# Three fused stages on one core: pack of attention in two parts, W' emptied by ScalarE and stored per batch, join reordered with four early steps

## The reference

```python
batch, n_heads, seq, head_dim = (8, 8, 576, 64); n_pack = 32
p_packed = sm_attn(p, k, v)              # softmax attention of 32 rows p over 576 keys, per head
out = sm_attn(q, p_packed, p_packed)     # softmax attention of 576 rows q over the 32 packed rows
x = out.transpose(0, 2, 1, 3).reshape(4608, 512)
h = x @ w_in                             # 512 -> 2048
P = a[0] + a[1]*h + a[2]*h**2 + a[3]*h**3
Q = 1.0 + abs(b[0])*abs(h) + abs(b[1])*h**2
y = (P / (Q + 1e-6)) @ w_out             # 2048 -> 512
h = y @ w_in2                            # 512 -> 1024
solu = h * softmax(h)
ln = (solu - mean) / sqrt(var + 1e-6) * g_ln
return ln @ w_out2                       # 1024 -> 512
```

## Time and profile before

| | us |
|---|---|
| median of three runs (lowest, highest) | 1328.96 (1325.56, 1330.09) |
| the profiled execution, its own time | 1329.48 |
| its span in the profile | 1327.3 |
| attention without jobs, until | 79.9 |
| attention with jobs, until | 207 |
| join, until | 263.6 |
| rational stage, until about | 885 |
| last stage, until the end | 1327 |

### The profile page before, as it was taken

How to read it: one execution, slowest core, us unless ns; L and a number is a source line. 1 busy time by engine, 2 the same in 40 slices (tenths; PEclk the granted TensorE clock), 3 DMA queues, 4 the chain that set the end, 5 groups by cost and what they waited for, 6 DMA issues and landing times.

```text
span 1327.3 us, 27768 instructions
## 1 busy us (share of the span) xinstructions
PE 1221.9 (92%) x10944; PEld 1095.7 (83%) x10944; DVE 1009.8 (76%) x1694; ACT 862.3 (65%) x1406; POOL 306.9 (23%) x205
## 2 busy tenths in 40 slices
PE   5678776599999999999999999999999999999999
PEld 3455554499999999999999999998888888888887
DVE  3657666599999999999999999986555555555553
ACT  3345435489989899999999999974344343433433
POOL 2222222033323232333332333331110111001100
PEclk8899888699999999999999999999999999999999
DMA  7668865402121121211212121111111111111110
GB/s 267 218 232 313 283 225 187 161 26 75 43 67 43 42 75 44 66 59 36 66 60 75 38 73 40 36 35 51 48 47 32 47 47 47 46 33 47 47 33 32
DMA packets 69790, 114.28 MB, mean 86 GB/s; under 512 B 9264, under 2 KB 39984, under 8 KB 69680
## 3 DMA queue, kind: packets, MB, share of 16 engines
q1 hardware_dynamic: 69680, 112.75, 26.1%
HBM read 72.36 MB, written 40.37 MB: 85 GB/s over the span
## 4 chain that ended last, share of the span: by engine, by line
PE 46%; DVE 29%; issue 14%; ACT 11%; DMA 0%; POOL 0%; ACTq 0%; SPq 0%; DVEq 0%
DVE num L989 6%; DVE rec L986 6%; PE ps_h L72 6%; PE ps_h L74 6%; PE ps_h L73 6%; PE ps_o L72 5%; PE ps_o L74 5%; PE ps_o L73 5%; DVE den L978 4%; ACT rec L898 3%; DVE num L973 3%; PE ps_s L359 3%; ACT rec L901 3%; PE ps_t L1231 2%; PE ps_s L347 2%
## 5 line engine op out<-in xcount | busy, mean ns | idle before, releaser
L72 PE MATMUL ps_y<-g_hi,wout_hi 128*128 128x288 f32 x1024 | 306.7, 299 | 16.7 <-ACT y_out L930 16.7
L940 POOL TENSOR_TENSOR den<-den,h_abs 128x576 f32<-128x576 f32 x128 | 203.0, 1586 | 458.5 <-ACT den L893 458.5
L73 PE MATMUL ps_y<-g_lo,wout_hi 128*128 128x288 f32 x1024 | 304.7, 298 | 0.0
L74 PE MATMUL ps_y<-g_hi,wout_lo 128*128 128x288 f32 x1024 | 303.8, 297 | 0.0
L72 PEld LDWEIGHTS ps_y<-g_hi,wout_hi 128*128 128x128 f32 x1024 | 194.5, 190 | 19.9 <-issue 19.8
L74 PEld LDWEIGHTS ps_y<-g_hi,wout_lo 128*128 128x128 f32 x1024 | 195.3, 191 | 0.0
L73 PEld LDWEIGHTS ps_y<-g_lo,wout_hi 128*128 128x128 f32 x1024 | 194.8, 190 | 0.0
L72 PE MATMUL ps_h<-x_hi,wp_hi 128*128 128x288 f32 x512 | 154.7, 302 | 10.5 <-DVE wp_lo L955 10.5
L73 PE MATMUL ps_h<-x_lo,wp_hi 128*128 128x288 f32 x512 | 153.4, 300 | 0.0
L74 PE MATMUL ps_h<-x_hi,wp_lo 128*128 128x288 f32 x512 | 152.7, 298 | 0.0
L893 ACT ACTIVATE den<-h_abs,kept 128x576 f32<-128x576 f32 x128 | 111.4, 870 | 38.4 <-DVE rec L986 38.3
(11 more groups left out here) (120 smaller groups left out, 2623.1 us busy)
## 6 DMA issues: line engine op xcount, KB each, us to landing
wp_scratch<-wp_out SPq DMA_DIRECT2D x32, 512.0 KB, 4.0
wp_lo<-wp_scratch SPq DMA_DIRECT2D x128, 128.0 KB, 3.0
k_main<-in_k SPq DMA_DIRECT2D x16, 576.0 KB, 6.4
q_main<-in_q SPq DMA_DIRECT2D x16, 576.0 KB, 6.7
v_main<-in_v SPq DMA_DIRECT2D x16, 576.0 KB, 5.7
y_scratch<-y_out SPq DMA_DIRECT2D x16, 576.0 KB, 3.3
y_lo<-y_scratch SPq DMA_DIRECT2D x36, 256.0 KB, 3.0
out<-result SPq DMA_DIRECT2D x36, 256.0 KB, 2.1
```

Of the source, the lines that this page charges most:

```text
L72: pe.matmul(out, lh, rh, start=first, stop=False)
L73: pe.matmul(out, lh, rl, start=False, stop=False)
L74: return pe.matmul(out, ll, rh, start=False, stop=last)
L940: pool.tensor_tensor(den[s % 2][:, :, :], den[s % 2][:, :, :], h_abs[s % 2][:, :, :], ALU.mult)\
```

## The change

Six things are changed. The pack is issued in two halves with the transposes of q between them. Of the scores of q only the last of nine tiles waits for the low half of the packed transpose. Of the first 12 jobs, ACT empties both heads of a block in one instruction of 1024 elements, and DVE none; the last four jobs are shared as before. `wp_scratch` is laid out by batch, so that a store of 128 rows goes to four places of 32 rows, and a load of a block is one transfer of 128 rows in place of four of 32. The orders on ACT and DVE inside an iteration are changed (ACT splits the next weights ahead of the second exponential, DVE does the sums ahead of the normalised pack and turns the keys ahead of the low half). The join is reordered and holds four steps of the rational stage in place of three. The diff, cut to what is spoken of:

```diff
@@ -269,15 +273,16 @@
 
     def store_job(sp, m):
         quad, a, half = job_parts(m)
-        for r, ready in enumerate((wp_act_out, wp_dve_out)):
-            sp.wait_ge(ready, 2 * m + 2)
-            sp.dma_start(wp_d[quad, 2 * a + r, :, half * 2 * BLOCK:(half + 1) * 2 * BLOCK],
+        sp.wait_ge(wp_act_out, 2 * m + 2)
+        wait_for(sp, wp_dve_out, dve_blocks(m + 1))
+        for r in range(2):
+            sp.dma_start(wp_d[QUAD * quad:QUAD * (quad + 1), 2 * a + r, :, half * 2 * BLOCK:(half + 1) * 2 * BLOCK],
                          wp_out[m % 2][:, r, :, :].rearrange("p n f -> p (n f)")).then_inc(wp_stored[m % 2][r], 16)
 
     def store_a2(sp, i):
         bt, g = group_at(i)
         sp.wait_ge(a2_ready, i + 1)
-        sp.dma_start(a2_d[HEAD_TILES * bt + g], a2_out[i % 2][:, :]).then_inc(a2_stored[bt // QUAD], 16)
...
@@ -349,16 +354,18 @@
                                        start=(b == 0), stop=(b == DB - 1), skip_group_check=True)
             mm.then_inc(s1_done, 1)
 
-        def pack(pe, i):
-            pe.wait_ge(probs1T_ready, i + 1)
-            pe.wait_ge(v_in[i % 2], 16 * (i // 2 + 1))
-            wait_for(pe, shift2_ready, i)
-            wait_for(pe, packT4_lo_ready, i)
-            for t in range(RUN):
+        def pack(pe, i, half):
+            if half == 0:
+                pe.wait_ge(probs1T_ready, i + 1)
+                pe.wait_ge(v_in[i % 2], 16 * (i // 2 + 1))
+                wait_for(pe, shift2_ready, i)
+                wait_for(pe, packT4_lo_ready, i)
+            for t in range(half * PAIRS, (half + 1) * PAIRS):
                 for h in range(GH):
                     mm = pe.matmul(ps_pack[head(h), :], probs1T[head(h), t, :], v_main[i % 2][head(h), t, :],
                                    start=(t == 0), stop=(t == RUN - 1), skip_group_check=True)
-            mm.then_inc(pack_done, 1)
+            if half == 1:
+                mm.then_inc(pack_done, 1)
 
         def turn_queries(pe, i):
             pe.wait_ge(q_in[i % 2], 16 * (i // 2 + 1))
...
@@ -379,9 +385,10 @@
 
         def scores_of_q(pe, i):
             pe.wait_ge(packT2_out, i + 1)
-            pe.wait_ge(packT4_lo_ready, i + 1)
             pe.wait_ge(qT_out, i + 1)
             for j in range(PAIRS):
+                if j == PAIRS - 1:
+                    pe.wait_ge(packT4_lo_ready, i + 1)
                 for h in range(GH):
                     mm = pe.matmul(scores2[head(h), j * 2 * PACK:(j + 1) * 2 * PACK], qT[i % 2][:, j, head(h)],
...
@@ -408,33 +414,36 @@
         scores_of_packed(pe, 0)
         for i in range(GROUPS):
             if i >= 1:
-                pack(pe, i - 1)
+                pack(pe, i - 1, 0)
             turn_queries(pe, i)
             if i >= 1:
-                turn_packed(pe, i - 1)
+                pack(pe, i - 1, 1)
             job_block(pe, i, 0)
             if i >= 1:
+                turn_packed(pe, i - 1)
+            job_block(pe, i, 1)
+            if i >= 1:
                 scores_of_q(pe, i - 1)
-            job_block(pe, i, 1)
             if i + 1 < GROUPS:
                 scores_of_packed(pe, i + 1)
 
         last = GROUPS - 1
-        pack(pe, last)
+        pack(pe, last, 0)
+        pack(pe, last, 1)
         job_block(pe, GROUPS, 0)
-        turn_packed(pe, last)
         pe.wait_ge(exp1_ready, GROUPS)
         features(pe, 0)
+        turn_packed(pe, last)
+        job_block(pe, GROUPS, 1)
         scores_of_q(pe, last)
-        job_block(pe, GROUPS, 1)
+        pe.wait_ge(wp_act_out, 2 * job_at(GROUPS) + 1)
+        features(pe, 1)
         a, b, c, d = range(JOBS - LAST_JOBS, JOBS)
         last_job_block(pe, a, 0)
-        features(pe, 1)
+        features(pe, 2)
         last_job_block(pe, a, 1)
-        last_job_block(pe, b, 0)
-        last_job_block(pe, b, 1)
-        features(pe, 2)
-        for m in (c, d):
+        features(pe, 3)
+        for m in (b, c, d):
             for n in range(2):
                 last_job_block(pe, m, n)
 
...
+                wait_for(act, wp_stored[m % 2][1], 16 * (m // 2))
+                act.activation(wp_out[m % 2][:, :, n, :], ps_turn[:, 2 * n:2 * n + 2, :], ACT.Copy)\
+                    .then_inc(wp_act_out, 1)
+            else:
+                act.activation(wp_out[m % 2][:, 0, n, :], job_bank(m, n, 0), ACT.Copy).then_inc(wp_act_out, 1)
+
+        weights_high(act, 0)
         for i in range(GROUPS):
-            weights_high(act, i)
             first_terms(act, i)
             last_pair_to_sbuf(act, i)
+            qT_to_sbuf(act, i)
             if i == 1:
                 act.wait_ge(zeros, 1)
             if i >= 1:
                 packT_to_sbuf(act, i - 1)
-            qT_to_sbuf(act, i)
             if job_at(i) is not None:
                 job_to_sbuf(act, job_at(i), 0)
+                job_to_sbuf(act, job_at(i), 1)
+            if i + 1 < GROUPS:
+                weights_high(act, i + 1)
+            else:
+                next_coefficients(act)
+                first_splits(act)
             if i >= 1:
                 second_terms(act, i - 1)
-            if job_at(i) is not None:
-                job_to_sbuf(act, job_at(i), 1)
 
         last = GROUPS - 1
-        next_coefficients(act)
-        first_splits(act)
+        a, b, c, d = range(JOBS - LAST_JOBS, JOBS)
         job_to_sbuf(act, job_at(GROUPS), 0)
+        step(act, 0)
         packT_to_sbuf(act, last)
-        step(act, 0)
+        job_to_sbuf(act, job_at(GROUPS), 1)
         second_terms(act, last)
-        job_to_sbuf(act, job_at(GROUPS), 1)
-        a, b, c, d = range(JOBS - LAST_JOBS, JOBS)
+        step(act, 1)
         job_to_sbuf(act, a, 0)
-        step(act, 1)
         job_to_sbuf(act, a, 1)
         job_to_sbuf(act, b, 0)
+        step(act, 2)
         job_to_sbuf(act, b, 1)
-        step(act, 2)
-        for m in (c, d):
-            for n in range(2):
-                job_to_sbuf(act, m, n)
+        job_to_sbuf(act, c, 0)
+        step(act, 3)
...
@@ -597,47 +615,43 @@
         turn_keys(dve, 0)
         for i in range(GROUPS):
             row_max(dve, i)
+            if i >= 2:
+                second_sums(dve, i - 2)
             if i >= 1:
                 normalized_pack(dve, i - 1)
-            if i >= 2:
-                second_sums(dve, i - 2)
             turn_probs1(dve, i)
+            if i + 1 < GROUPS:
+                turn_keys(dve, i + 1)
             if i >= 1:
                 packT_low(dve, i - 1)
-            if i + 1 < GROUPS:
-                turn_keys(dve, i + 1)
             if i >= 2:
                 turn_probs2(dve, i - 2)
-            if job_at(i) is not None:
-                job_to_sbuf(dve, job_at(i), 0)
             if i >= 1:
                 shifted_scores(dve, i - 1)
-            if job_at(i) is not None:
-                job_to_sbuf(dve, job_at(i), 1)
 
         last = GROUPS - 1
-        normalized_pack(dve, last)
-        second_sums(dve, last - 1)
+        a, b, c, d = range(JOBS - LAST_JOBS, JOBS)
         next_coefficients(dve)
         first_splits(dve)
-        job_to_sbuf(dve, job_at(GROUPS), 0)
+        second_sums(dve, last - 1)
+        normalized_pack(dve, last)
+        step(dve, 0)
         packT_low(dve, last)
         turn_probs2(dve, last - 1)
-        step(dve, 0)
         shifted_scores(dve, last)
-        job_to_sbuf(dve, job_at(GROUPS), 1)
-        a, b, c, d = range(JOBS - LAST_JOBS, JOBS)
+        step(dve, 1)
         job_to_sbuf(dve, a, 0)
         second_sums(dve, last)
-        step(dve, 1)
         job_to_sbuf(dve, a, 1)
+        job_to_sbuf(dve, b, 0)
+        step(dve, 2)
         turn_probs2(dve, last)
-        job_to_sbuf(dve, b, 0)
         job_to_sbuf(dve, b, 1)
-        step(dve, 2)
-        for m in (c, d):
-            for n in range(2):
-                job_to_sbuf(dve, m, n)
+        job_to_sbuf(dve, c, 0)
+        step(dve, 3)
+        job_to_sbuf(dve, c, 1)
+        job_to_sbuf(dve, d, 0)
+        job_to_sbuf(dve, d, 1)
 
     def gpsimd(pool, step):
...
+    EARLY = 4
...
@@ -762,19 +776,18 @@
 
     def load_x(sp, q):
         bt, half = q // 2, q % 2
-        sp.wait_ge(attention["a2_stored"][0 if q == 0 else 1], 16 * HEAD_TILES * QUAD)
+        for stored in attention["a2_stored"][0 if q == 0 else 1]:
+            sp.wait_ge(stored, 16 * QUAD)
         sp.dma_start(x_raw(q), a2_d[HEAD_TILES * bt:HEAD_TILES * (bt + 1), :, half * CHUNK:(half + 1) * CHUNK]
                      .rearrange("g p n -> p g n")).then_inc(x_in[q % 2], 16)
 
     def load_block(sp, bt, n):
-        quad, at = bt // QUAD, (bt % QUAD) * PACK
+        quad = bt // QUAD
         for stored in attention["wp_stored"]:
             for r in range(2):
                 sp.wait_ge(stored[r], 16 * (JOBS // 4) * (quad + 1))
-        for h in range(GH):
-            sp.dma_start(block_raw(n)[h * PACK:(h + 1) * PACK, :, :],
-                         wp_d[quad, h:HEADS:GH, at:at + PACK, n * BLOCK:(n + 1) * BLOCK].rearrange("g r f -> r g f"))\
```

(58 more changed lines are left out.)

1 line of the change is left out of this document (removed).

## The result

The changed kernel takes **1365.8 us** (median of 4 runs, 1365.09 to 1367.45) where the kernel before takes 1328.56: 37 us slower, ratio 1.0285, 95% interval 1.0264 to 1.0305. The profiled execution took 1365.09 us, 35.6 more than that of before.

A forecast was written before the change was run, and what follows sets the result against it. Before 263.6 us a ring of waits bounds the loop, with DMA close behind; the changed stores, on four engines, become the bound. 1329.5 + 34.8 (first x) + 9.1 (join), about +44, gives 1373.5 us; range 1340 to 1412.

The forecast's parts named there:

- Stores on four engines: Stores of W': each, cut 4 x 32, was to run on four of 16 DMA engines at 25.0 GB/s each.
- First x +34.8 us: Job loop: 4.12 MB on each of four engines delays the rational stage's first split of x by 34.8 us.
- Join +9.1 us: Join: the second x, queued behind the last stores, is split 71.7 us after the first instead of 62.6.
- Low half only at the last tile: Scores of q on PE: waiting for the low half only at the last tile costs nothing and gives nothing.
- The other parts, -4 in the loop and -7 in the join, hidden: Loop and join: reordering gains 4 us and 7 us, hidden while the stores of W' come last.
- The DVE chain of 1.78 us: Job iterations: one copy (0.61 us) and the second softmax sums (1.17 us) leave DVE's 7.6 us chain.
- the transposes' 1.03 us: Job iterations: nine transposes of q inside the pack delay its end by 1.03 us.
- The weights' 4 us: Job loop: ACT's earlier wait for weights takes half of the remaining 0.75 us gain per iteration, leaving 4 us.
- A: Rival, stores of W': they run on 16 engines as before, giving 1318.5 us; chance 0.12.
- B: Rival, stores of W': four engines at about 30 GB/s each, loss and gain cancel, 1328 us; chance 0.03.
- C: Rival, stores of W': four engines at 28.2 GB/s each throughout, giving 1347 us; chance 0.05.
- D: Rival, job loop: waits for the single weights buffer do not overlap transfers, iterations 18.2 us, total 1385 us; chance 0.10.

The follow-up runs named there:

- e2: The kernel before with only the new layout of W' (stores cut 4 x 32, one-piece block loads, attention output semaphores per buffer): 1369.16 us, ratio 1.0314.
- e1: The changed kernel with the old layout of W' (stores of 128 rows outermost, block loads in four pieces), all other parts kept: 1315.65 us, ratio 0.9908.
- e3: The changed kernel with its layout by batch, but each store of W' issued as four pieces of 32 rows: 1313.36 us, ratio 0.9892.
- m1: Transfers only, 512 KB one at a time in several shapes, no kernel: 128 rows 2.6 us, 4 x 32 10.0 us, four pieces of 32 rows 3.5 us.
- e8: e1 with the scores of q waiting for the low half of the pack ahead of their first tile again: 1327.74 us, ratio 0.9995.
- e7: e1 with DVE's old order (second softmax sums behind the normalised pack, keys turned behind the low half): 1319.29 us, ratio 0.9925.
- e12: e1 with the W' blocks of the eleven jobs inside the loop emptied by ACT and DVE in halves again: 1313.25 us, ratio 0.9886.
- e5: e1 with the pack in one piece again, ahead of the transposes of q: 1311.21 us, ratio 0.9873.
- e6: e1 with the weights split by ACT at the start of an iteration again, behind the second exponential: 1312.43 us, ratio 0.9881.
- e9: e1 with three early steps, step 3 of the rational stage behind the jobs again: 1318.67 us, ratio 0.9929.
- e10: e3 with the first of each job's two stores as one transfer cut 4 x 32 again: 1327.85 us, ratio 1.0001.

## Why the prediction was right, point by point

*Stores on four engines: right.* e2 and e1 show that this part makes the loss, e3 that the counting does and not the address, m1 the four engines. The Trainium skill's rule on the slowest dimension ("DMA: Bandwidth & Descriptors", section "Why a DMA increments its semaphore by 16 and not by 1") gives 4 for this store, and the traces agree: four small packets for a store of 4 x 32, a share of 0.2 and some 100 GB/s where only stores of 4 x 32 are left, 0.90 and 298 GB/s with pieces of 32 rows.

*First x +34.8 us: right in kind, 9.3 too high.* Measured +25.5. Two terms of the product were off. The first store is issued at 75.85 us instead of 81.14, because the light iterations became shorter. The 4.12 MB then land in about 161 us instead of 164.9: 25.6 GB/s per engine over the stretch where I took 25.0 (26.1 in a steady iteration, which takes 16.3 us where 17.0 were forecast). The isolated store was the right row to take, its highest slot (28.2) and the share among 16 (21.0) were not. The "~27 GiB/s" of the Trainium skill, in the table at the head of "DMA: Bandwidth & Descriptors" (29.0 GB/s), is more than the 26.1 of the steady iteration.

*Join +9.1 us: right.* From split to split 73.56 us against the 71.7 of the working, +10.95, with ACT waiting for the second x as forecast, 12.42 us. The sum is 7.7 us too high (1373.5 against 1365.8), mostly by the first term; that this one is 1.9 us too low hides a part of it.

*Low half only at the last tile, "costs nothing and gives nothing": wrong.* It was judged from VectorE's rows alone. The wait stood on PE, 1.7 us before the scores in a light iteration of before. The clock of that run of scores is the last shown under e8:

```profile
62.39 2.15 PE L386 MATMUL ps_s<-packT,qT 128*32 128x64 f32 x72 [1.70 <-issue]
```

e8 shows 12 us for it. By the seventh copy of the queries, the last one before the job iterations settle, 9.2 us of them are there (86.38 us in e8, 77.16 in e1, 88.17 in the kernel before). For the light iterations the prediction had put the other parts at nothing too. It came out right all the same because the stores hide this gain but for the 5.3 us by which they start earlier.

*The other parts, -4 in the loop and -7 in the join, hidden:* the sum of 11 is near the 12.5 us of e1, but it is made of other terms, and the nearness is luck. In e1's trace 11.0 us are gained by the seventh copy of the queries; from there to the last copy e1 takes 116.1 us where the kernel before takes 114.0, so the job iterations, forecast at -4, gain nothing. The DVE chain of 1.78 us an iteration (e7 and e12 gave +3.6 and -2.4 where 17.8 were summed) is worth little, and the transposes' 1.03 us less than said (e5: -4.4 where -10 was forecast, and not told from no change); the likely reason, not tried by itself, is that the job iterations wait for transfers too (share 0.90 in e3). The weights' 4 us (e6: 3.2) and the early step's 4 us (e9: 3.0) fit, without being told from no change. From split to split the join takes 59.2 us in e1, 3.4 less than before; 1.5 us more come from the negation (ACT waits 1.41 us for it where the earlier trace rows have 2.92).

*Rivals.* A's time, 1318.5, is near that of e1 and e3 (1315.7 and 1313.4), where the stores are on 16 engines. Its 188.7 us are those in which the changed kernel would equal the one before; with 11 us gained they would be 177.7, at 32.7 GB/s for each of the four. B (30.8 GB/s) and C (28.2) are out by the 25.6 measured. D is out: its chain of weights is the one that the profile names, but the period is 16.3, not 18.2, and e2 has the same period with the old order on ACT; the share never fell under that of four engines, so the queues did not run dry. A chain of waits names who is served last, not what is full: here the weights wait behind the stores on the same four engines.

*Signs.* Stores landing after 10 us or more (14.12 in the join), late loads, ACT and DVE waiting and iterations near 17 us all came; the mean share was 0.66 and not 0.5, and why the other twelve were busy for longer was not looked into.

Left open: why e3's profiled execution, at 1307.16, is faster than its other runs (1312.66 to 1315.21), whether the small differences among e5, e6 and e12 are real, and what sets TensorE's clock in the light iterations.

## What to carry to other kernels

Before a layout in DRAM is changed, count the outermost entries on both sides of each transfer: a store of 128 rows cut 4 x 32 ran on four engines and cost 50 us here, and four transfers of 32 rows to the same addresses ran on all 16. When transfers bind, look at the share in narrow slots and at the bytes on the fullest engine, not at the mean. And price a removed wait on the engine that waits, in every kind of iteration and not only in the one under study.

## What the runs showed of the hardware

- A store on four engines, alone, is slower than four engines in a filled queue: m1's 4 x 32 carries 53 GB/s with the gaps between transfers, while the slots of the changed kernel's join in which only four engines are busy mostly read 93 to 114 GB/s, with more stores queued behind. The slots of one such store, 0.25 us each:

```profile
GB/s 0 0 0 49 49 49 49 66 33 66 98 66 66 33 49 16 0 82 49 33 82 66 66 66 82 98 115 66 131 82 66 49 49 66 33 66 49 16 0 0
```

- 16 x 8 rows need 3.7 us where 128 rows need 2.6, although both can feed 16 engines; what takes the rest isn't shown.
- The issues of SP take longer where stores on four engines stand ahead of them. The issue of k, right behind a pair of stores, takes 3.24 us (median) and 3.23 in e2, against 0.79 before, 1.35 in e1 with the same orders and 0.80 in e10, where one store in two runs on four engines. What holds it is not shown. Rows (instructions on the tile k_main, duration ns min/median/max, after and before):

```profile
L257 SPq DMA_DIRECT2D k_main<-in_k x7: 3232/3237/4564, 89.9 to 189.4; - x7
```

```profile
L253 SPq DMA_DIRECT2D k_main<-in_k x7: 432/786/1968, 96.8 to 170.9; - x7
```

- Pieces cost issues: in e3 the eight stores of a job take SP 4.7 to 6.2 us from the first issue to the end of the last, where two took 0.8 us before (1.9 once). e3 is no slower than e1 for it.
